# Folding token blocks straight from the accumulation bank, ahead of ScalarE's copy

## What is computed

```python
for b in range(nb):                                # attention, by blocks of tokens
    intra = (qb @ kb.T * Dmask) @ vb
    inter = (qb * lam_pow) @ kv_state
    out[:, :, sl] = intra + inter
    kv_state = lam_block * kv_state + kb_dec.T @ vb
x = out in (B=2, S=768, 512)
X = np.fft.fft(np.fft.fft(x, axis=1), axis=2)      # sequence, then features
u = x + np.real(X)
u = u + relu(layernorm(u) @ w_ch1) @ w_ch2         # first layer
out = u + relu(layernorm(u) * g @ w_ch1b) @ w_ch2b # second layer
```

## Time and profile before

| | us |
|---|---|
| median of 3 runs (lowest, highest) | 624.18 (623.84, 625.25) |
| the profiled execution, whole | 626.46 |
| its span in the trace | 624.5 |
| TensorE busy in the span | 597.9 |
| VectorE busy | 371.2 |
| ScalarE busy | 242.4 |
| GpSimd busy | 152.7 |

### The profile page before, as it was taken

One profiled execution on the slowest core, in us unless ns is written; L12 is line 12 of the kernel. 1 busy time (PEld: TensorE's weight loads), 2 busy tenths in 40 slices (PEclk: granted clock), 3 DMA queues, 4 the chain that ended last, 5 costly groups with the idle time before them and its releaser, 6 DMA issues.

```text
span 624.5 us, 10866 instructions
## 1 busy us (share of the span) xinstructions
PE 597.9 (96%) x4143; PEld 407.7 (65%) x4143; DVE 371.2 (59%) x637; ACT 242.4 (39%) x488; POOL 152.7 (24%) x133
## 2 busy tenths in 40 slices
PE   8999899978989999999999999999999999999997
PEld 4898656745666666666666666576666666666664
DVE  2569948967678586556676888733345334433223
ACT  0332143643465432443356675234422344232231
POOL 1547644833532000110322763001000010000000
PEclk9999699979999999999999999999999999999999
DMA  8999780000000263331123231100001000010001
GB/s 243 392 382 382 274 243 1 1 2 1 0 2 1 76 162 102 101 102 44 60 68 99 71 116 54 34 2 1 1 26 44 1 2 1 0 68 1 1 2 68
DMA packets 41412, 50.43 MB, mean 81 GB/s; under 512 B 2442, under 2 KB 28690, under 8 KB 39956
## 3 DMA queue, kind: packets, MB, share of 16 engines
q1 hardware_dynamic: 39156, 45.05, 21.9%
q10 hardware_dynamic: 1728, 3.15, 1.3%
q0 software_dynamic: 480, 1.57, 0.9%
HBM read 43.46 MB, written 6.30 MB: 80 GB/s over the span
## 4 chain that ended last, share of the span: by engine, by line
PE 66%; DVE 11%; POOL 7%; issue 7%; DMA 5%; ACT 3%; SPq 1%; DVEq 0%; ACTq 0%; POOLq 0%
PE bank L572 30%; PE bank L552 26%; PE bank L472 4%; DMA arena<-attn 3%; PE bank L409 2%; DMA arena<-w 1%; PE bank L404 1%; DVE arena L1034 1%; PE bank L541 1%; POOL arena L1410 1%; DVE arena L1042 1%; DVE arena L1035 1%; DVE arena L1155 1%; POOL arena L1357 1%; POOL arena L1354 1%
## 5 line engine op out<-in xcount | busy, mean ns | idle before, releaser
L572 PE MATMUL bank<-arena 128*128 128x512 f16 x1152 | 288.2, 380 | 2.9 <-DVE arena L1163 2.0
L552 PE MATMUL bank<-arena 128*128 128x256 f16 x2016 | 262.6, 275 | 9.6 <-DVE arena L1204 6.7
L552 PEld LDWEIGHTS bank<-arena 128*128 128x128 f16 x2016 | 198.2, 99 | 85.0 <-DVE arena L1204 7.6
L572 PEld LDWEIGHTS bank<-arena 128*128 128x128 f16 x1152 | 112.7, 98 | 90.2 <-DVE arena L1163 2.6
L1155 DVE SCALAR_TENSOR_TENSOR arena<-arena 128x512 f16<-128x512 f32 x96 | 71.1, 741 | 76.4 <-ACT arena L804 76.3
L804 ACT ACTIVATE arena<-arena 128x512 f16<-128x512 f32 x96 | 60.4, 629 | 101.0 <-DVE arena L1204 95.6
L1198 DVE SCALAR_TENSOR_TENSOR arena<-bank,arena 128x256 f32<-128x256 f32 x48 | 20.2, 422 | 71.8 <-PE bank L552 71.8
L1367 POOL TENSOR_TENSOR arena<-arena 128x512 f32<-128x512 f32 x6 | 8.3, 1379 | 150.9 <-ACT arena L775 90.8
L1149 DVE TENSOR_TENSOR arena<-arena 128x512 f16<-128x512 f32 x42 | 35.5, 855 | 12.2 <-ACT arena L788 12.2
L859 ACT ACTIVATE arena<-bank 128x256 f32<-128x256 f32 x48 | 18.3, 382 | 58.2 <-PE bank L552 58.2
L968 DVE TENSOR_REDUCE arena<-arena 128x1 f32<-128x1024 f32 x32 | 38.3, 1209 | 0.0
(11 more groups left out here) (97 smaller groups left out, 556.7 us busy)
## 6 DMA issues: line engine op xcount, KB each, us to landing
arena<-w SPq DMA_DIRECT2D x48, 256.0 KB, 4.5
arena<-w SPq DMA_DIRECT2D x24, 512.0 KB, 3.8
arena<-attn SPq DMA_DIRECT2D x10, 1024.0 KB, 8.8
x_dram<-arena ACTq DMA_DIRECT2D x12, 256.0 KB, 6.5
out<-arena SPq DMA_DIRECT2D x12, 256.0 KB, 2.1
arena<-attn SPq DMA_DIRECT2D x4, 512.0 KB, 4.3
arena<-c SPq DMA_DIRECT2D x1, 1153.5 KB, 11.0
arena<-g SPq DMA_DIRECT2D x1, 514.0 KB, 12.6
```

Source lines behind the costliest of these rows:

```text
L552: last = nc.tensor.matmul(bank_, wst[:, i, wx, w, kt, :], xs[s % 2][:, ux, x, kt, :], start=not started and k == 0, stop=k == 5, skip_grou ...
L572: last = nc.tensor.matmul(ops[t][:], hT[n % 2][:, half, hx, t * P:(t + 1) * P], wdn[:, i, wx, half * DM:(half + 1) * DM], start=first and ...
```

## The change

`fold_tokens` waits for the matmuls of the unit (`pv_done`) instead of for ScalarE's copy (`x_done`), and reads the second-half block from the bank `xps[b]` instead of from SBUF. Since two engines are not to read a bank at once, ScalarE's copy of units 6 to 11 waits in turn for the fold (`sf_done`). In these units ScalarE does `expand` ahead of `x_rows`, and `expand` waits for the matmuls of the unit too. The four maxima of the first matrix's chunks 4 to 7 move from iterations 8 to 11 of VectorE's loop to behind the loop. On TensorE the first three groups of the sequence transform run their products c = 0 and 1 first, six in all, and then the three products c = 2, which alone wait for `fold_last`.

```diff
+            def first_sequence():
+                pe.wait_ge(fold_done[0], HALF - 1)
+                for f in range(3):
+                    for c in range(HALF - 1):
+                        along(f, c)
+                for f in range(3):
+                    pe.wait_ge(fold_last, 1 + f // 2)
+                    along(f, HALF - 1).then_inc(f1_done, 1)
...
-            sequence(range(4))
+            first_sequence()
+            sequence(range(3, 4))
...
                 act.wait_ge(pv_done, u + 1)
+                if c >= HALF:
+                    act.wait_ge(sf_done, u - B * HALF + 1)
                 rows_u = xlow[:, b, c, :] if c < HALF else xhigh[:, c - HALF, b, :]
...
+                act.wait_ge(pv_done, u + 1)
                 act.wait_ge(st_done, u + 1)
...
             for u in range(UNITS):
-                x_rows(u)
-                if u < UNITS - B:
+                if u < B * HALF:
+                    x_rows(u)
                     expand(u)
+                else:
+                    if u < UNITS - B:
+                        expand(u)
+                    x_rows(u)
...
                 c, b = divmod(u, B)
-                dve.wait_ge(x_done, u + 1)
+                dve.wait_ge(pv_done, u + 1)
...
-                lo, hi = xlow[:, b, c - HALF, :], xhigh[:, c - HALF, b, :]
+                lo, hi = xlow[:, b, c - HALF, :], xps[b][:]
                 nc.vector.tensor_tensor(to[:, b, 0, :], lo, hi, ALU.add)
                 nc.vector.tensor_tensor(to[:, b, 1, :], lo, hi, ALU.subtract).then_inc(sf_done, 1)
...
-                if UNITS - SLOTS <= u < UNITS:
-                    largest(0, u - UNITS + SLOTS)
+                if 2 * B <= u < 2 * B + SLOTS // 2:
+                    largest(0, u - 2 * B)
+            for c in range(SLOTS // 2, SLOTS):
+                largest(0, c)
```

More of the change, by code:

```diff
@@ L451, in _, with along @@
             pe.wait_ge(mask_done, 2 * UNITS)
+            def along(f, c):
+                b, par, dk = f // 8, f // 4 % 2, f % 4
+                n = NE if par == 0 else NO
+                lhs = fold[:, b, 2 * par + dk // 2, c, (dk % 2) * P:(dk % 2 + 1) * P]
+                return nc.tensor.matmul(f1_bank[f % 3][:, 0:n], lhs, C1[:, c, par * NE:par * NE + n],
+                                        start=c == 0, stop=c == HALF - 1)
+            def first_sequence():
[6 more added lines that the diff above has]
+                    along(f, HALF - 1).then_inc(f1_done, 1)
             def sequence(groups):
                 for f in groups:
[L456 to L463, removed]
+                    b = f // 8
                     if f == 8:
@@ L468, in sequence @@
                         pe.wait_ge(y_done, f - 2)
-                    n = NE if par == 0 else NO
                     for c in range(HALF):
-                        lhs = fold[:, b, 2 * par + dk // 2, c, (dk % 2) * P:(dk % 2 + 1) * P]
-                        last = nc.tensor.matmul(f1_bank[f % 3][:, 0:n], lhs, C1[:, c, par * NE:par * NE + n],
-                                                start=c == 0, stop=c == HALF - 1)
+                        last = along(f, c)
                     last.then_inc(f1_done, 1)
```

## The result

The changed kernel took 618.0 us (median of 4, 616.28 to 619.58) against 624.48 (median of 4, 623.84 to 625.25): a ratio of 0.9895, 95% interval 0.9861 to 0.9929, faster by 6.5 us. Forecast were 616.1 and a gain of 8.1, with a range of 614.6 to 620.3; 618.0 is inside it, but 0.2 above the forecast's own part of it (614.6 to 617.8). That is more than the medians show, and the experiments explain part of it. In what follows, one of the 47 executions of before that were run beside the experiments, 633.36 us, counts as slow and is left out.

What follows compares the result with a forecast made beforehand. VectorE was taken to set TensorE's pace from 54 to 66 us. Waits (0.2 + 1.0 + 2.84) and clock (2.29 + 1.88), together 8.21, less 0.1 for late maxima, gave 8.1: 624.18 to 616.1 us, range 614.6 to 620.3.

Steps and rivals of the forecast that it cites:

- the forecast's own part of it: Range of the main forecast without rival 1: 614.6 to 617.8 us, chance 0.71.
- VectorE's pace: From 54 to 66 us VectorE sets the pace; with the change 3.4 us per unit against TensorE's some 4.5.
- The price of a fold from the bank: Two instructions per new fold in VectorE's loop, 1.28 us together, priced by the mask's row of 674 to 692 ns.
- My rival of a bank-sourced fold held up by GpSimd: Bank folds in VectorE's loop take up to 2.03 us per instruction: 2.4 us slower, 626.6 us; chance 0.04.
- The waits: TensorE, up to unit 11's rows: 0.2 at GpSimd's scaling, 1.0 before unit 10's rows, 2.84 before unit 11's.
- the term of 0.2: GpSimd's instruction at 48.33 us takes 1.91 instead of 2.12 us, since VectorE's decay comes earlier.
- The clock term: TensorE's clock stays up: 2.29 us saved in unit 11's rows and 1.88 in the sequence transform's groups 0 to 3.
- the same shift gives 624.18 - 8.1 = 616.1: The runs' median lies 2.3 us below the profiled execution and was taken to gain the same 8.1 us.
- My rival 1: TensorE gets its lower clock near 65 us all the same; only waits of 4.0 us saved, 620.1 us; chance 0.15.
- The early products: Sequence transform on TensorE: without the reorder it would wait up to 1.6 us for the folds, with it none.
- The moved maxima: Behind VectorE's loop they fit with 0.7 us at the first maximum, about nothing at `tops`; 0.1 us taken off.
- my sign of being wrong: At TensorE's L525: a wait on VectorE of more than half a microsecond would show the forecast wrong.

Runs made afterwards that it cites:

- gpsimd_held: Kernel before, with GpSimd's feature folds held until VectorE's fold of unit 9 is over: 624.98 us against 623.89, ratio 1.0011.
- late_bank: Kernel before with only the fold's operand moved to the bank; the fold still waits for ScalarE's copy: 617.13 us against 624.97, ratio 0.9886.
- before_both_fills: Kernel before, with useless matmuls in TensorE's wait before unit 11's rows and its idle time near 125 us: 619.09 us against 624.78, ratio 0.9913.
- bank_only_filled: Changed kernel with maxima and sequence transform in their old places, plus 36 useless matmuls in TensorE's idle 4.3 us: 614.5 us against 624.78, ratio 0.9845.
- filled_wait: Kernel before, with three useless 512-column matmuls between the rows of units 10 and 11: 622.14 us against 623.89, ratio 0.9959.
- changed_again: The changed kernel measured once more, on another chip, against the kernel before: 616.62 us against 624.97, ratio 0.9874.
- old_sequence: Changed kernel with the sequence transform in its old order, without the early products: 617.52 us against the kernel before's 624.97, ratio 0.9883.
- bank_only: Changed kernel with the four maxima and the sequence transform put back in their old places: 617.11 us against the kernel before's 623.89, ratio 0.9881.
- maxima_only: Kernel before with only the four maxima moved behind VectorE's loop; folds still read SBUF: 622.22 us against 623.89, ratio 0.9993.
- filled_second: Changed kernel with 36 useless short matmuls in TensorE's idle 4.3 us at 116 to 120 us: 614.94 us against the kernel before's 624.97, ratio 0.9850.

## Why the prediction was right, and where a term was off

**VectorE's pace, and why.** Right. The price of a fold from the bank, 0.67 to 0.69 us, is what the mask's row gave. `gpsimd_held` and `late_bank` show from two sides that the operand freed it from GpSimd. No surcharge for the bank was seen: 673 to 689 ns, against 0.68 and 0.69 us in SBUF without GpSimd, and two in a row start 0.60 or 0.61 us apart with either operand. By that the larger fixed part for PSUM sources in the Trainium skill, VectorE: DVE Perf Modes, the TRN2 errata, doesn't hold for this instruction, which has one source in a bank and one in SBUF. My rival of a bank-sourced fold held up by GpSimd has no support: all 12 instructions took 0.67 to 0.69, and ten of them started during one of GpSimd's.

**The waits.** Forecast 0.2 + 1.0 + 2.84 = 4.0; `before_both_fills` against `bank_only_filled` gives 4.6. In the changed trace unit 10's rows start 1.63 us earlier (60.69 less 59.06) where 1.2 were forecast, since the keys' and values' matmuls start at 50.00 instead of 50.57. Of this 0.57, GpSimd's L1332 at its lone 1.91 us is the 0.2 forecast, and the rest is a load that landed earlier (GpSimd starts at 47.96 instead of 48.32). Neither is the change's doing. `filled_wait` and `before_both_fills` have VectorE's old order and start at 47.70 and 48.06, and the instruction takes 1.91 in both. So the term of 0.2 was an accident of the profiled execution, and the waits proper were forecast at 3.84 where 4.6 were measured (4.5 between the two traces: second `spread_back` at 91.17 and 86.72).

**The clock term.** Right for the profiled execution, and not borne out for the median. The forecast took 2.29 + 1.88 = 4.2 us off the profiled execution, and the traces bear that out: 5.15 us for unit 11's rows became 2.68 (64.47 less 61.79), and 10.16 for the first 24 matmuls became 7.98, together 4.65 (0.3 of the excess, since 8.28 had been taken for the 24). But `filled_wait` has the term alone, and there the median gained 1.75 (2.6 by the ratio, 4.1 at most). So the step that doesn't hold as written is "the same shift gives 624.18 - 8.1 = 616.1": an execution of before with a low mean clock (0.984, 626.46 us, 2.3 above the median) was taken as shifted as a whole, while the median execution had less clock to lose. How much less in this stretch isn't shown. The two errors, waits too low and clock too high, have opposite signs, so that the sum came as near as it did is partly luck. It did not come out too high everywhere: forecast and median gain differ by 1.6 us in the first comparison, inside what the scatter allows, and `changed_again` gained 8.35, a little more than forecast. Ten executions of the changed kernel in the two comparisons have a median of 616.8.

**My rival 1**, that the clock doesn't follow, was wrong as a mechanism: the stretch is at 1.00 in every trace of the change. Its figure of 620.1 is near `before_both_fills` by chance only.

**The early products.** I wrote that TensorE would wait up to 1.6 us without them. That was an error of my own arithmetic: groups 0 and 1 need only the first `fold_last`, forecast at 65.1, and take 4 us, behind which the second, at 66.8, is long there. `old_sequence` waited 0.16 us.

**The moved maxima.** The tie at the first `spread_back` came as forecast (my sign of being wrong, more than half a microsecond at L525, was meant for it; the second one waits 1.09 us as it waited 1.08 before): 0.24 us of wait in the changed kernel, 0.27 in `changed_again`, none in `bank_only`, where VectorE waits 1.53 us for TensorE instead. In this stretch the move costs a little and gives nothing, once the folds are short; ahead of that (`maxima_only`) it is eaten by a decay that then meets GpSimd.

## What to carry to other kernels

When an elementwise instruction on VectorE takes twice its time now and then, lay GpSimd's timeline beside it: two SBUF inputs meet GpSimd's, one input left in its bank does not, and that one operand was worth more here than reordering around the slow instruction. Before an execution's low clock is booked as a gain, compare its mean clock with those of the other executions, and count only what the median one has. Before two traces are subtracted, look for what differs ahead of the edited code, such as a load that landed half a microsecond earlier. Test the parts of a change singly: three of the four edits here could not be told from nothing.

## What the runs showed of the hardware

- A VectorE instruction with two SBUF inputs that starts during a GpSimd instruction with two inputs ends about 0.55 us after it at 128x512 (62.17 to 63.92 us against 63.37), and 0.28 after it at 128x256 (54.75 to 55.45 against 55.17 in the changed kernel). At 128x512 it takes 0.68 us alone, and from 0.82 (`late_bank`) to 1.77 (`maxima_only`) when met, by how much of GpSimd's was left; GpSimd's own goes from 1.27 to 1.72. The same shape with one input in PSUM stays at 0.67 to 0.69.
- In the profile of before, the clock fell to 1.2 GHz towards the end of an idle time of 2.85 us. TensorE then worked from 66.39 to about 76 before it was back at 2.4 GHz. Behind the idle time at 116 to 120 us it was back within 4 us of work in `changed_again` (0.60 and 0.55 in the stretches from 120 to 124, 1.00 from 124).
- The same idle time is not always followed by a fall. One of 2.36 to 2.38 us, near 145 us in the changed kernel and somewhat later in the kernel before, was followed by a stretch at 1.2 GHz in 8 traces and by none in 4 (`bank_only`, `late_bank`, `changed_again`, `filled_second`). Idle times of 1.06, 1.71 and 1.24 us one after the other (`maxima_only`, 59 to 69 us) left it up.
- One kernel's executions on one core each, on three chips, lie between 621.0 and 629.1 us, ordered by mean granted clock. Filling two idle times with useless matmuls gained 5.7 us (624.78 to 619.09) without shortening any wait.
